# Attention with top-k masks and two expert layers: the sums and inverses of a round two rounds on, and the divides between the mask subtractions

## The chip, the cores and the metric

The kernel runs on one core of a Trainium2 chip. It uses five engines that run side by side: TensorE (PE in the profile, with its weight loads as PEld), VectorE (DVE), ScalarE (ACT), GpSimd (POOL), and SyncE (SP), which issues most DMAs. The metric is the device time of one execution in microseconds, lower is better.

## The reference

Three parts follow one another. Attention has 4 batches, 8 heads, 576 positions and head size 64. In it only the 32 largest scores of each row count. The second part is a layer of three projections whose elementwise maximum is projected back. The third sends each of the 2304 tokens to one of 8 experts.

```python
scores = scale * np.matmul(q, k.transpose(0, 1, 3, 2))
kth = np.partition(scores, -32, axis=-1)[..., -32:-31]
scores = np.where(scores >= kth, scores, -1e9)
attn = np.exp(scores - scores.max(-1, keepdims=True))
attn = attn / (attn.sum(-1, keepdims=True) + 1e-9)
x = np.matmul(attn, v)                                  # then tokens x 512
x = np.maximum(np.maximum(x @ w1, x @ w2), x @ w3) @ w_out
logits = x @ w_gate + modality_bias[modality_id]        # one expert per token
out = gate_w * (np.maximum(x @ w1[e], 0) @ w2[e])       # for the tokens of expert e
```

## The kernel before

Attention runs in 48 rounds. A round takes one pair of heads and a block of 192 queries, as three tiles of 128 rows (tiles 0 and 1 are one head each, tile 2 holds the remaining 64 rows of both). Each engine has its own program, a loop over rounds, and waits on semaphores that count the steps of the others. All queues are in order.

What happens to round r, engine by engine:
- TensorE computes its scores two rounds early, in its own round r-2: items Q0, Q1, Q2 (`score_tile`, L1324 and L1329). It transposes the probabilities in its round r+2: items H0, H1, H2 (`transpose_tile`, L1342). It multiplies them with the values in round r+3: item V (`weigh_values`, L1358). Between these stand the matmul groups of the second part (`moe_group`). The order inside a round comes from `round_items`: Q0, V, Q1, H0, half of the groups, H1, Q2, H2, the other groups. Which groups fall into which round is written out in `PARTS`, a cycle of eight rounds (one for 384 tokens), in use from round 6 on; rounds 2 to 5 have one group each that multiplies weights. Round 16 is the third of a cycle, and has a transposing group and two small products for the gate.
- ScalarE copies the scores out (`copy_scores`, L938 to L946). When `kth` is there, it makes a mask for each tile (`under`, L919, writing `below`): those of tiles 0 and 1 near the end of its round r, that of tile 2 behind the copy of Q0 in round r+1. In round r+1 it takes the exponentials and their row sums (`exp`, L927), and in round r+2 copies the transposed probabilities (`copy_probsT`, L956).
- VectorE selects the 32 largest in its round r: a chain of seven steps k = 0 to 6 of MAX8 and MATCH_REPLACE8 for each tile (L1130, L1132), and at the end `kth` (L1172). In the midst of this chain of round r it adds the sums of round r-1 (`full_sums`, L1115, behind step 5) and inverts them (`inverses`, L1120, in step 6).
- GpSimd, in its round r: subtracts the masks of round r-1 from the scores, three tiles (`leave_out`, L787); adds the two ways of the second part where a unit is finished (`add_ways`, L818); makes the key differences for round r+3 (L729); folds the scores of round r+2 (L740 to L743); multiplies the exponentials of round r-1 by the inverse sums, three tiles (`divide`, L795); and in the first rounds subtracts weights (L809).

The exponential of a tile waits for its subtraction (`masked_ready`). The transpose of a tile waits for its divide (`probs_ready`). `divide(r)` waits for `inverses(r)`.

The buffers: the probabilities and the sums have two slots, by r % 2. The scores have four, and `below` has one for each tile.

After the last round come the remaining groups. Then the tokens are listed and gathered by expert, and the experts' products follow (L1450, L1467) from about 748 us on.

Of the kernel before, what the change touches and what calls it, by code (L numbers as in the profile page):

```python
# [27 lines left out]
ROUNDS = BLOCKS * RPB  # L28
# [4 lines left out]
GROUP = 3  # L33
# [21 lines left out]
FOLDED = 2  # L55
FOLD_BUFS = 3

AFTER_Q0, AFTER_H0, AFTER_H2, AHEAD_OF_LAST = 0, 3, 7, 9
INVERSE_AT = 5
TOP_BUFS = 3  # L60
CHAIN_STEPS = CHAIN * GROUP + SMALL_CHAIN * FOLDED

# [40 lines left out]
def wait_apart(eng, passed, sem, value):  # L103


    eng.wait_ge(sem, value)
    eng.sem_inc(passed, 1)
# [53 lines left out]
def scored(r, i):  # L161


    return r * GROUP + score_order(r).index(i) + 1


def in_range(r):

    return 0 <= r < ROUNDS


def finished_units(r):

    return [(m, g[1]) for m, g in maxout_groups(r) if g[0] == "A" and g[2] == WAYS - 1]
# [227 lines left out]
def program(nc, qT, kT, v, w_in, w3T, w_out, w_gate, modality, bias, e_w1, e_w2, shared, x2_dram, list_dram, out):  # L402

    with ExitStack() as ctx:
# [311 lines left out]
        def _(pool):  # L716
# [5 lines left out]
            def key_differences(r):  # L722

                slot = r % 2
                pool.wait_ge(qk_in[slot], (r // 2 + 1) * QK_LOADS)
                if r >= 2:

                    wait_apart(pool, passed, scores_ready, scored(r - 2, 1))
                nc.gpsimd.tensor_tensor(k_diff[:, slot, :], k_sb[:, slot, 0:HALF], k_sb[:, slot, HALF:SEQ],  # L729
                                        ALU.subtract).then_inc(k_diff_ready, 1)  # L730

            def fold(r):

                slot, ring = r % FOLD_BUFS, r % RING
                wait_apart(pool, passed, scores_copied, scored(r, 1))
                if r >= FOLD_BUFS:

                    wait_apart(pool, passed, topk_step, (r - FOLD_BUFS + 1) * CHAIN_STEPS)
                second = scores[:, ring, 0:FOLDED, HALF:SEQ]
                nc.gpsimd.tensor_tensor(upper[:, slot, :, :], second, rise[:, :, :], ALU.add).then_inc(fold_step, 1)  # L740
                nc.gpsimd.tensor_tensor(lower[:, slot, :, :], second, fall[:, :, :], ALU.subtract).then_inc(fold_step, 1)  # L741
                pool.wait_ge(fold_step, r * 3 + 1)
                nc.gpsimd.tensor_tensor(scores[:, ring, 0:FOLDED, 0:HALF], upper[:, slot, :, :], fall[:, :, :],  # L743
                                        ALU.subtract).then_inc(fold_step, 1)
# [34 lines left out]
            nc.gpsimd.memset(shared.places[:, :, 1:ENTRY], 0.0)  # L779
            nc.gpsimd.iota(shared.places[:, :, 0:1].bitcast(I32), [[P, T], [0, 1]], base=0, channel_multiplier=1)  # L780

            def leave_out(r):

                for i in range(GROUP):

                    wait_apart(pool, passed, below_ready, r * GROUP + i + 1)
                    nc.gpsimd.tensor_tensor(scores[:, r % RING, i, :], scores[:, r % RING, i, :], below[:, i, :],  # L787
                                            ALU.subtract).then_inc(masked_ready, 1)

            def divide(r):  # L790

                pool.wait_ge(inverses_ready, r + 1)
                for i in range(GROUP):
                    part = probs[:, r % PROB_BUFS, i, 0:SEQ]
                    nc.gpsimd.tensor_scalar(part, part, inverse[:, r % 2, i:i + 1], 0.0, ALU.mult, ALU.add)\  # L795
                      .then_inc(probs_ready, 1)

            def weight_difference(n):

                w, c = n // DK, n % DK  # L800
                if n == 0:
                    pool.wait_ge(w_in_sem, 16 * WAYS)
                if n == DK:
                    pool.wait_ge(w3_in_sem, 16 * 2)
                if w == 1:

                    pool.wait_ge(w_differences, c + 1)
                other = w_sb[:, 1, c, :] if w == 0 else w3_sb[:, c, :]
                nc.gpsimd.tensor_tensor(w_sb[:, w, c, :], w_sb[:, w, c, :], other, ALU.subtract)\  # L809
                  .then_inc(w_differences, 1)  # L810

            def add_ways(m, u):

                n, half, first = m * UNITS + u, u // HALF_UNITS, u % HALF_UNITS * 2

                pool.wait_ge(moe_copied, PLACE[m, ("A", u, 1)] + 1)
                both = [ways[:, n % UNIT_BUFS, w, :].rearrange("p (a n) -> p a n", a=2) for w in range(WAYS)]
                nc.gpsimd.tensor_tensor(hT[:, m % 2, first:first + 2, half * BLK:(half + 1) * BLK], both[0], both[1],  # L818
                                        ALU.add).then_inc(ways_added, 1)

            for r in range(-AHEAD, LOAD_AT + 1):
                if in_range(r - 1):
                    leave_out(r - 1)
                for m, u in finished_units(r - 1):
                    add_ways(m, u)
                if in_range(r + AHEAD + 1):
                    key_differences(r + AHEAD + 1)
                if in_range(r + AHEAD):
                    fold(r + AHEAD)
                if in_range(r - 1):  # L830
                    divide(r - 1)
                if r + AHEAD < DK * WAYS:
                    weight_difference(r + AHEAD)

# [67 lines left out]
        def _(act):  # L902
# [99 lines left out]
            def one_round(r):  # L1002
# [29 lines left out]
                for _, step in steps[ran:]:  # L1032
                    step()
# [76 lines left out]
        def _(dve):  # L1110
            def full_sums(r):


                dve.wait_ge(exps_done, (r + 1) * GROUP)
                nc.vector.tensor_reduce(full_sum[:, r % 2, :], sums[:, r % 2, :, :], AX.X, ALU.add).then_inc(sum_step, 1)  # L1115

            def inverses(r):

                dve.wait_ge(sum_step, r + 1)
                nc.vector.reciprocal(inverse[:, r % 2, :], full_sum[:, r % 2, :]).then_inc(inverses_ready, 1)  # L1120

            def one_round(r):
                slot, steps = r % FOLD_BUFS, [r * CHAIN_STEPS]

                def select(k, src, dst, best, before):

                    if k > 0:
                        wait_apart(dve, passed, topk_step, before)
                    if k % 2 == 0:
                        nc.vector.max(best, src).then_inc(topk_step, 1)  # L1130
                    else:
                        nc.vector.match_replace(dst, best, src, LOWEST).then_inc(topk_step, 1)  # L1132
                    steps[0] += 1
                    return steps[0]

                def full(k, before):
                    if k == 0:

                        wait_apart(dve, passed, scores_copied, scored(r, FOLDED))
                    return select(k, scores[:, r % RING, FOLDED, :] if k < 2 else work[:, :], work[:, :],  # L1140
                                  best_eight(r, FOLDED, k // 2), before)

                upper_at, lower_at, full_at = [0] * FOLDED, [0] * FOLDED, 0
                if r == 0:
                    for k in range(CHAIN):
                        full_at = full(k, full_at)
                for k in range(CHAIN):
                    if k < 2:

                        wait_apart(dve, passed, fold_step, r * 3 + (1 if k == 0 else 3))  # L1150
                    for i in range(FOLDED):
                        part = upper[:, slot, i, :]
                        upper_at[i] = select(k, part, part, best_eight(r, i, k // 2), upper_at[i])
                        if k == INVERSE_AT + 1 and i == 0 and r >= 1:
                            inverses(r - 1)
                    if r > 0:
                        full_at = full(k, full_at)
                    if k == 0:

                        wait_apart(dve, passed, fold_step, r * 3 + 2)  # L1160
                    for i in range(FOLDED if k < SMALL_CHAIN else 0):
                        part = lower[:, slot, i, :]
                        lower_at[i] = select(k, part, part, best_eight_lower(r, i, k // 2), lower_at[i])
                    if k == INVERSE_AT and r >= 1:
                        full_sums(r - 1)

                wait_apart(dve, passed, topk_step, steps[0])
                pairs = top[:, r % TOP_BUFS, :, 0:TOP_STEP * (TOPK // 2 + 1)]
                nc.vector.tensor_reduce(smaller[:, :, :], pairs.rearrange("p i (j a) -> p i j a", a=TOP_STEP),
                                        AX.X, ALU.min).then_inc(pair_step, 1)  # L1170
                dve.wait_ge(pair_step, r + 1)
                nc.vector.tensor_reduce(kth[:, r % TOP_BUFS, :], smaller[:, :, :], AX.X, ALU.max).then_inc(kth_ready, 1)  # L1172
# [2 lines left out]
            dve.wait_ge(sum_pads_ready, 1)  # L1175
            for r in range(ROUNDS):
                one_round(r)


            link = linker(dve, early.step)  # L1180
            dve.wait_ge(ids_in, 16)
# [372 lines left out]
```

## Time and profile before

| | us |
|---|---|
| median of 3 runs | 968.61 (967.39 to 971.51) |
| the profiled execution | 970.57 |
| its span, from first to last instruction | 969.0 |
| TensorE busy (matmuls) | 908.8 |
| VectorE busy | 717.8 |
| GpSimd busy | 660.3 |
| ScalarE busy | 577.4 |
| mean granted TensorE clock | 0.990 |

A busy time is the sum over the engine's instructions. An engine that is idle waits for a semaphore, and the profile names the instruction that released it. In a timeline a row merges instructions of one line that follow one another: start in us, time in us, engine, line, operation, output and inputs, count. In brackets stands how long the engine was idle ahead of it, and for whom. Two instructions of one engine overlap a little at their ends, so a row of three is shorter than three times one.

Rounds can be told apart by TensorE's rows: each begins with Q0 (L1324 from `k_sb`), and H0 is the first row of L1342 behind the second row of L1324 (from `k_diff`).

### The profile page before, as it was taken

How to read it: one execution, taken by the hardware profiler on the slowest of the kernel's cores; microseconds unless marked ns; L12 is line 12 of the kernel's file. 1: busy time of each engine (PE TensorE's matmuls, PEld its weight loads, DVE VectorE, ACT ScalarE, POOL GpSimd, SP SyncE). 2: the span in 40 equal slices, each digit the busy share in tenths (PEclk: the TensorE clock that was granted, in tenths of full speed). 3: DMA queues.
4: the chain of work that ended last, by engine and by line, in shares of the span. 5: the costliest groups of instructions: out<-in, count | busy, mean ns of one | idle time of the engine just before them, and what ended most of it. 6: DMA issues, size and time to landing. Idle time of an engine off the chain costs nothing.

```text
span 969.0 us, 17781 instructions
## 1 busy us (share of the span) xinstructions
PE 908.8 (94%) x5132; PEld 690.2 (71%) x5133; DVE 717.8 (74%) x2191; ACT 577.4 (60%) x1226; POOL 660.3 (68%) x624
## 2 busy tenths in 40 slices
PE   4688999999999999999999999999999999999996
PEld 2354857768585776758586685957685998998895
DVE  5999999989999989999999899999503621251120
ACT  2577786777777777767777677776523321342211
POOL 7999997887988789888878879885453312231221
PEclk9999998999999999999999999999999999999998
DMA  5821121232211222121112222111043061116110
GB/s 196 253 58 46 42 59 57 58 113 55 60 44 56 68 58 67 44 68 51 49 58 57 63 58 60 53 30 46 13 145 100 18 221 56 54 38 222 43 54 32
DMA packets 69270, 70.84 MB, mean 73 GB/s; under 512 B 15456, under 2 KB 50560, under 8 KB 69184
## 3 DMA queue, kind: packets, MB, share of 16 engines
q1 hardware_dynamic: 65264, 59.44, 20.2%
q0 software_dynamic: 3920, 10.40, 3.5%
q8 instruction: 36, 0.59, 0.2%
q14 instruction: 50, 0.41, 0.1%
HBM read 59.05 MB, written 10.76 MB: 72 GB/s over the span
## 4 chain that ended last, share of the span: by engine, by line
PE 71%; issue 10%; ACT 6%; DVE 5%; POOL 3%; DMA 1%; POOLq 0%; SPq 0%; DVEq 0%; ACTq 0%
PE m_ps L1385 17%; PE m_ps L1467 10%; PE s_ps L1450 8%; PE t_ps L1342 7%; PE m_ps L1411 7%; PE o_ps L1358 5%; PE m_ps L1399 5%; PE s_ps L1324 4%; PE s_ps L1329 3%; PE o_ps L1450 3%; DVE top L1130 2%; ACT probs L927 1%; POOL dispatch_list L395 1%; PE m_ps L1418 1%; PE m_ps L1404 1%
## 5 line engine op out<-in xcount | busy, mean ns | idle before, releaser
L787 POOL TENSOR_TENSOR scores<-scores,below 128x576 f32<-128x576 f32 x144 | 200.3, 1417 | 88.0 <-ACT below L919 87.4
L1385 PE MATMUL m_ps<-xT,w_sb 128*128 128x192 f32 x1152 | 199.6, 331 | 1.2 <-ACT xT L963 1.2
L1385 PEld LDWEIGHTS m_ps<-xT,w_sb 128*128 128x128 f32 x1152 | 189.8, 193 | 1.5 <-ACT xT L963 1.5
L1130 DVE MAX8 top<-upper 128x8 f32<-128x288 f32 x384 | 159.4, 448 | 0.7 <-issue 0.6
L1132 DVE MATCH_REPLACE8 upper<-top,upper 128x288 f32<-128x288 f32 x288 | 125.3, 443 | 0.2 <-issue 0.2
L1342 PEld LDWEIGHTS t_ps<-ident,probs 128*128 128x128 f32 x720 | 80.3, 142 | 59.6 <-issue 51.1
L927 ACT ACTIVATE probs<-scores,shift 128x576 f32<-128x576 f32 x144 | 111.3, 783 | 18.3 <-issue 18.3
L956 ACT COPY probsT<-t_ps 128x640 f32<-128x640 f32 x192 | 103.4, 564 | 28.0 <-PE t_ps L1342 26.8
L1342 PE MATMUL t_ps<-ident,probs 128*128 128x128 f32 x720 | 107.4, 280 | 11.8 <-ACT probsT L956 11.8
L795 POOL TENSOR_SCALAR probs<-probs,inverse 128x576 f32<-128x576 f32 x144 | 105.4, 754 | 7.3 <-DVE inverse L1120 7.2
L919 ACT ACTIVATE below<-scores,steep_kth 128x576 f32<-128x576 f32 x144 | 106.6, 771 | 2.2
L1130 DVE MAX8 top<-work 128x8 f32<-128x576 f32 x144 | 107.1, 744 | 0.4
L864 POOL DMA_INDIRECT out_rows<-y_sb,info x18 | 17.9, 997 | 109.0 <-ACT y_sb L1056 71.9
L1358 PE MATMUL o_ps<-probsT,v_sb 128*64 128x192 f32 x960 | 88.6, 331 | 1.9 <-issue 1.5
L1411 PE MATMUL m_ps<-wo_sb,stage 128*128 128x512 f32 x192 | 85.2, 592 | 0.0
L1358 PEld LDWEIGHTS o_ps<-probsT,v_sb 128*64 128x64 f32 x960 | 65.9, 136 | 26.4 <-issue 20.2
L984 ACT ACTIVATE stage<-m_ps 128x384 f32<-128x384 f32 x72 | 35.2, 489 | 74.7 <-PE m_ps L1385 74.7
L1130 DVE MAX8 top<-lower 128x8 f32<-128x288 f32 x192 | 77.2, 445 | 0.5 <-POOL lower L741 0.5
L740 POOL TENSOR_TENSOR upper<-scores,rise 128x576 f32<-128x576 f32 x48 | 67.9, 1415 | 5.7 <-ACT fall L944 5.2
L1216 DVE SCALAR_TENSOR_TENSOR hTl<-s_ps,hTh 128x384 fp32r<-128x384 f32 x36 | 19.8, 556 | 70.1 <-ACT hTh L1048 70.1
L1132 DVE MATCH_REPLACE8 work<-top,work 128x576 f32<-128x576 f32 x96 | 71.3, 742 | 0.0
L1329 PE MATMUL s_ps<-k_sb,q_rest 128*128 128x288 f32 x192 | 59.0, 433 | 10.8 <-ACT fall L944 6.0
(208 smaller groups left out, 1789.1 us busy)
## 6 DMA issues: line engine op xcount, KB each, us to landing
k_sb<-keys_t SPq DMA_DIRECT2D x48, 288.0 KB, 2.6
v_sb<-values SPq DMA_DIRECT2D x48, 256.0 KB, 2.7
raw<-e_w SPq DMA_DIRECT2D x12, 1024.0 KB, 5.4
maxout_rows<-x_rows SPq DMA_DIRECT2D x18, 256.0 KB, 2.2
q_sb<-queries_t SPq DMA_DIRECT2D x48, 64.0 KB, 2.5
w_sb<-w SPq DMA_DIRECT2D x2, 1536.0 KB, 8.3
q_rest<-queries_t SPq DMA_DIRECT2D x96, 16.0 KB, 2.3
v_sb<-values SPq DMA_DIRECT2D x48, 32.0 KB, 2.6
```

The lines of the kernel that those rows point to most:

```text
L787: nc.gpsimd.tensor_tensor(scores[:, r % RING, i, :], scores[:, r % RING, i, :], below[:, i, :], ALU.subtract).then_inc(masked_ready, 1)
L795: nc.gpsimd.tensor_scalar(part, part, inverse[:, r % 2, i:i + 1], 0.0, ALU.mult, ALU.add)\
L919: nc.scalar.activation(below[:, i, :], scores[:, r % RING, i, :], ACT.Relu, bias=steep_kth[:, top_slot, i:i + 1], scale=-STEEP).then_inc(b ...
L927: nc.scalar.activation(probs[:, r % PROB_BUFS, i, 0:SEQ], scores[:, r % RING, i, :], ACT.Exp, bias=shift[:, top_slot, i:i + 1], scale=SCAL ...
L956: ins = nc.scalar.copy(probsT[:, h, :, row:row + rows], blocks[:, :, part:part + rows])
L1130: nc.vector.max(best, src).then_inc(topk_step, 1)
L1132: nc.vector.match_replace(dst, best, src, LOWEST).then_inc(topk_step, 1)
L1342: ins = nc.tensor.transpose(t_ps[:, c * P:(c + 1) * P], probs[:, r % PROB_BUFS, i, c * P:(c + 1) * P], ident[:, :])
L1358: ins = nc.tensor.matmul(o_ps[h * HEAD:(h + 1) * HEAD, 0:BLK], v_sb[:, slot, c, h * HEAD:(h + 1) * HEAD], probsT[:, h, c, :], start=(c == ...
L1385: ins = nc.tensor.matmul(dst[:, a * BLK:(a + 1) * BLK], w_sb[:, w, c, (first + a) * P:(first + a + 1) * P], xT[:, m % 2, c, b % SPAN * BLK ...
L1411: ins = nc.tensor.matmul(dst[:, :], hT[:, m % 2, j, i * P:(i + 1) * P], wo_sb[:, j, :], start=False, stop=(j == FB - 1))
L1450: ins = nc.tensor.matmul(h_ps[f % H_BANKS][:, 0:CH], w[:, k, f * P:(f + 1) * P], x[:, k, :], start=(k == 0 and i == 0), stop=(k == DK - 1 ...
```

## The change

VectorE takes the sums of round r-2 behind step 0 of round r and inverts them in step 1, instead of those of round r-1 in steps 5 and 6. The sums and inverses of the last round but one follow behind the loop. GpSimd divides round r-2 in its round r, between the subtractions of tiles 0 and 1 and that of tile 2, instead of dividing round r-1 at the end of round r.

```diff
-            def leave_out(r):
-                for i in range(GROUP):
+            def leave_out(r, tiles):
+                for i in tiles:
                     wait_apart(pool, passed, below_ready, r * GROUP + i + 1)
...
             for r in range(-AHEAD, LOAD_AT + 1):
                 if in_range(r - 1):
-                    leave_out(r - 1)
+                    leave_out(r - 1, range(FOLDED))
+                if in_range(r - 2):
+                    divide(r - 2)
+                if in_range(r - 1):
+                    leave_out(r - 1, range(FOLDED, GROUP))
                 for m, u in finished_units(r - 1):
                     add_ways(m, u)
                 if in_range(r + AHEAD + 1):
                     key_differences(r + AHEAD + 1)
                 if in_range(r + AHEAD):
                     fold(r + AHEAD)
-                if in_range(r - 1):
-                    divide(r - 1)
...
                         upper_at[i] = select(k, part, part, best_eight(r, i, k // 2), upper_at[i])
-                        if k == INVERSE_AT + 1 and i == 0 and r >= 1:
-                            inverses(r - 1)
+                    if k == 1 and r >= 2:
+                        inverses(r - 2)
...
-                    if k == INVERSE_AT and r >= 1:
-                        full_sums(r - 1)
+                    if k == 0 and r >= 2:
+                        full_sums(r - 2)
...
             for r in range(ROUNDS):
                 one_round(r)
-
+            full_sums(ROUNDS - 2)
+            inverses(ROUNDS - 2)
```

`FOLDED` is 2 and `GROUP` is 3, so the first call takes tiles 0 and 1 and the second tile 2. The constant `INVERSE_AT` goes.

## Rows read from the trace of the kernel before

**Rows 1.** The page, part 1: busy us, share of the span and instructions.
```profile
PE 908.8 (94%) x5132; PEld 690.2 (71%) x5133; DVE 717.8 (74%) x2191; ACT 577.4 (60%) x1226; POOL 660.3 (68%) x624
```
**Rows 2.** List of waits: us in total, times, longest us.
```profile
POOL scores L787 <- ACT below L919: 87.4, 46, 4.9
...
DVE full_sum L1115 <- ACT probs L927: 26.7, 25, 2.9
...
ACT steep_kth L910 <- DVE kth L1172: 3.0, 4, 1.0
```
**Rows 3.** Timeline of GpSimd, rounds 16 to 22.
```profile
238.94 4.15 POOL L787 TENSOR_TENSOR scores<-scores,below 128x576 f32<-128x576 f32 x3 [3.89 <-ACT below L919]
...
249.87 2.17 POOL L795 TENSOR_SCALAR probs<-probs,inverse 128x576 f32<-128x576 f32 x3
...
264.65 4.15 POOL L787 TENSOR_TENSOR scores<-scores,below 128x576 f32<-128x576 f32 x3 [1.47 <-ACT below L919]
...
292.36 4.15 POOL L787 TENSOR_TENSOR scores<-scores,below 128x576 f32<-128x576 f32 x3 [1.99 <-ACT below L919]
...
306.53 4.25 POOL L787 TENSOR_TENSOR scores<-scores,below 128x576 f32<-128x576 f32 x3 [1.09 <-ACT below L919]
...
323.95 1.41 POOL L787 TENSOR_TENSOR scores<-scores,below 128x576 f32<-128x576 f32 x1 [2.61 <-ACT below L919]
```
**Rows 4.** Timeline of TensorE: item H0 of rounds 16, 18, 20 and 21.
```profile
241.42 0.76 PE L1342 MATMUL t_ps<-ident,probs 128*128 128x128 f32 x5
...
267.13 0.77 PE L1342 MATMUL t_ps<-ident,probs 128*128 128x128 f32 x5
...
295.64 0.77 PE L1342 MATMUL t_ps<-ident,probs 128*128 128x128 f32 x5
...
310.22 0.77 PE L1342 MATMUL t_ps<-ident,probs 128*128 128x128 f32 x5
```
**Rows 5.** Timeline of ScalarE: the third exponential of round 16.
```profile
244.38 0.80 ACT L927 ACTIVATE probs<-scores,shift 128x576 f32<-128x576 f32 x1
```
**Rows 6.** Timeline of GpSimd: the subtractions of rounds 2, 9 and 10.
```profile
46.55 4.15 POOL L787 TENSOR_TENSOR scores<-scores,below 128x576 f32<-128x576 f32 x3
...
136.75 4.16 POOL L787 TENSOR_TENSOR scores<-scores,below 128x576 f32<-128x576 f32 x3
...
149.25 4.14 POOL L787 TENSOR_TENSOR scores<-scores,below 128x576 f32<-128x576 f32 x3 [0.70 <-ACT below L919]
```
**Rows 7.** Timeline of TensorE: H0 of rounds 2, 6, 9; a wait; Q1 of 10.
```profile
43.75 1.33 PE L1342 MATMUL t_ps<-ident,probs 128*128 128x128 f32 x5
...
97.84 0.77 PE L1342 MATMUL t_ps<-ident,probs 128*128 128x128 f32 x5
...
100.83 4.49 PE L1385 MATMUL m_ps<-xT,w_sb 128*128 128x192 f32 x26 [1.23 <-ACT xT L963]
...
138.12 0.77 PE L1342 MATMUL t_ps<-ident,probs 128*128 128x128 f32 x5
...
151.03 0.76 PE L1324 MATMUL s_ps<-k_diff,q_sb 64*128 64x288 f32 x4 [1.94 <-ACT scores L938]
```
**Rows 8.** Timeline of ScalarE: an exponential of round 2, the scalars of round 9.
```profile
48.06 0.78 ACT L927 ACTIVATE probs<-scores,shift 128x576 f32<-128x576 f32 x1 [5.20 <-issue]
...
147.94 0.20 ACT L910 ACTIVATE steep_kth<-kth 128x3 f32<-128x3 f32 x1 [0.96 <-DVE kth L1172]
```
**Rows 9.** Timeline of VectorE: the sums in round 1.
```profile
37.54 0.16 DVE L1115 TENSOR_REDUCE full_sum<-sums 128x3 f32<-128x6 f32 x1 [1.80 <-ACT probs L927]
```
**Rows 10.** Timeline of GpSimd: the subtractions of round 48.
```profile
686.26 4.22 POOL L787 TENSOR_TENSOR scores<-scores,below 128x576 f32<-128x576 f32 x3 [4.94 <-ACT below L919]
```
**Rows 11.** Timeline of TensorE: item H0 of round 48.
```profile
689.00 0.77 PE L1342 MATMUL t_ps<-ident,probs 128*128 128x128 f32 x5
```
**Rows 12.** Busy us by stretch; PEclk is the granted clock, behind it DMA.
```profile
151.00:159.00 8.00, 7.96 (x33) 7.61 (x34) 8.00 (x25) 4.62 (x12) 7.24 (x6) 0.57 0.06 16
492.00:498.00 6.00, 6.00 (x33) 5.93 (x32) 5.90 (x19) 3.86 (x11) 6.00 (x6) 0.72 0.05 14
```

More of the change, by code:

```diff
@@ L58 @@
 AFTER_Q0, AFTER_H0, AFTER_H2, AHEAD_OF_LAST = 0, 3, 7, 9
-INVERSE_AT = 5
 TOP_BUFS = 3
```

## The prediction

> **What bounds the kernel now.** I read the page first, then the list of waits, then the timelines of GpSimd, TensorE and ScalarE side by side. The page gives TensorE 94% busy, VectorE 74%, GpSimd 68%, ScalarE 60% [rows 1]. The span has three parts. Up to about 147 us VectorE's selection, 13.35 us a round and almost without waits, and GpSimd's queue set the pace. From there to 709 us TensorE's own queue does: in most rounds its matmuls stand back to back. After that come the last projections and the experts, which the change does not touch.
>
> The waits that look like a prize are those of the edited lines: VectorE waits 26.7 us in 25 rounds at `full_sums` for the last exponential of the round before. GpSimd waits 87.4 us for ScalarE's masks ahead of its subtractions. But who waits for VectorE in turn? ScalarE waits for `kth` only 4 times, 3.0 us in all [rows 2]. A round of VectorE without its stall is 13.35 us; the eight TensorE rounds of a cycle (238 to 350 us) take 14.0 us each. So VectorE's stalls are slack it would otherwise spend elsewhere.
>
> **The change, part by part.** *Sums and inverses.* The same two small instructions a round stand at another place; they cost 0.16 us each in both [rows 9], so their work is priced at nothing. Their wait goes: in round r the exponentials of r-2 are long done. What is late next on VectorE is nothing that ScalarE waits for. The exception is the start: two stalls stand there, 1.80 us [rows 9] and one more of 1.1, and `kth` of rounds 3 to 9 comes 2.9 us earlier. This is worth something only where ScalarE waits for `kth`: 0.96 us in round 9 [rows 8].
>
> *Divides.* Before, `divide(r-1)` ends GpSimd's round r, and TensorE transposes its result in round r+1, several us later. In round 16 the three divides stand at 249.87 and take 2.17 us [rows 3]. After, `divide(r-2)` is issued in round r, behind the subtractions of tiles 0 and 1 of round r-1, and TensorE transposes it in the same round r (item H0, the fourth of the round). So H0 can start no sooner than the first subtraction plus two subtractions (4.15/3 = 1.38 us each, 2.77) plus one divide (2.17/3 = 0.72) plus the handover. For the handover I take 0.15: the first subtraction of rows 6 ends at 46.55 + 1.38 = 47.93 and ScalarE's exponential, which waited, starts at 48.06 [rows 6, 8]. Sum 3.65 us. The first subtraction itself waits for ScalarE's mask, which sits in ScalarE's queue near the end of TensorE's round before; so it cannot move ahead, and shifts with TensorE.
>
> That gives a test for each round: the distance from the first subtraction to H0 in the trace of before must be 3.65 us, or TensorE waits for the rest.
> - Round 16: 238.94 to 241.42, 2.48: short by 1.1 [rows 3, 4].
> - Round 17: its subtractions are bound by GpSimd's queue, whose total of work is the same; the shift of round 16 covers it: 0.
> - Round 18: 264.65 to 267.13, 2.48: short by 1.1 [rows 3, 4].
> - Round 20: 292.36 to 295.64, 3.28: short by 0.4 [rows 3, 4].
> - Round 21: 306.53 to 310.22, 3.69: just enough. Rounds 19 and 23 are like it or better [rows 3, 4].
> - Round 22: the divides fall into the 2.61 us in which GpSimd waits for the third mask [rows 3], 2.17 of work in 2.61 of waiting: hidden wholly. This is what the edit fits.
>
> So one cycle of eight rounds costs 1.1 + 1.1 + 0.4 = 2.6 us, and TensorE has no slack behind it to take it back. The cycle stands four times in full (rounds 16 to 47): 10.4 us. Round 12 has the distance of round 20: 0.4. Rounds 47 and 48 have too little as well: 686.26 to 689.00 [rows 10, 11] is short by 0.9, the other by 0.7: 1.6. Together 12.4.
>
> *The third subtraction* now comes 2.17 us later where no wait covers it, and ScalarE's third exponential waits for it. In round 16 that exponential started at 244.38 [rows 5]; now 238.94 + 4.15 + 2.17 = 245.26, 0.9 later, which is inside the 1.1 that H0 already costs. Behind it stand the copies that TensorE's H2 waits for, so if H0 were not late this would cost the 0.9 instead. The adds of the two ways, the key difference and the fold come 2.2 us later too; the fold of round 18 would end at 252, against ScalarE's next use of its buffers at 254.7: covered.
>
> *The start.* In round 2 the divides are no longer done at 43, ahead of the subtractions of 46.55, but behind two of them. GpSimd reaches these 2.2 us earlier (44.4), so the first divide ends at 47.9 and H0 of round 2 moves from 43.75 to 48.05: 4.3 us [rows 6, 7]. In rounds 3 to 6 a closed ring then runs: H0 and weight product 5.8, H1 and Q2 1.6, copy, scalars and mask 2.5, then the 3.65 above: 13.55 us a round, against (97.84 - 43.75)/4 = 13.5 before [rows 7]. So the 4.3 stays. Round 6 adds some 1.3 for a slower start-up of the first matmuls and the ring, and gives back 1.2, since TensorE's wait for `xT` goes [rows 7]: 4.3. Round 8 costs 0.4 more. In round 9 the subtractions are bound by GpSimd's queue: 136.75 + 4.3 + 3.65 = 144.7 against H0 at 138.12, 6.6, which is 2.0 more. In round 10 the 0.96 of `kth` is gained [rows 8], and 149.25 to H0 at 151.03 + 0.69 = 151.72, 2.47, is short by 1.2 [rows 6, 7]. Total of the start: 4.3 + 0.4 + 2.0 - 0.96 + 1.2 = 6.9. Its bounds: 0, if the waits that TensorE already has there absorb it, and 9.
>
> *The clock.* TensorE's granted clock averages 0.57 from 151 to 159 us [rows 12]: most of it at the lower of its two levels (1.2 of 2.4 GHz), just behind an idle time of 1.94 us [rows 7] and in a run of transposes and 8-column products. That costs 8.0 x 0.43 = 3.4 us. Round 34 has a fall of 6.0 x 0.28 = 1.7 us at the same place of the cycle [rows 12], behind a wait half as long; rounds 18, 26 and 42 have the same wait and no fall. The change adds 1.1 us idle exactly there. Bounds: nothing, or a fall of 3.4 in all four, 13.6 - 1.7 = 11.9 more than now. I take 3.4, one full fall more: the waits then come to 2.0 us together, which is near the row of 1.94, but only one of five such places has paid the full price.
>
> Sum: 12.4 + 6.9 + 3.4 = 22.7 us. The profiled execution took 970.57 us around a span of 969.0, 2 us above the median of 968.61. On it that is 993; on the median 991.
>
> **Rivals.** *A, the start is free.* TensorE waits often before 150 us, and VectorE comes 2.9 us earlier there. If the delay is absorbed and the clock stays as it is: 968.6 + 12.4 = 981. Against it: the waits in rounds 3 to 6 are waits for the same GpSimd queue.
>
> *B, the clock falls in every round like 18.* 968.6 + 12.4 + 6.9 + 11.9 = 1000. For it speaks round 10, against it rounds 26 and 42, which kept the clock.
>
> *C, the other side: VectorE's lead is passed on.* The mechanism is the removed wait at `full_sums` only: `kth` earlier, ScalarE's masks earlier, the subtractions earlier, and H0 covered. It decides from the point at which the first subtraction comes 1.2 us earlier in rounds 16 and 18. If only the start gains, 968.6 - 2.9 = 966; the whole 26.7 would make 942. Against it: ScalarE issues the mask in order, behind TensorE's last copies, and did not wait for `kth` there [rows 2]. A page of the Trainium skill would have it otherwise: Perfetto Trace Analysis, section "Identifying the Most-Contended Engine", says that matmul busy time is a poor measure, that TensorE is to be judged by weight loads, and that one should improve the engine with the highest occupancy. By that rule TensorE has 71%, VectorE 74% and is the one to free, and the change would gain. Rows 1 has both numbers; the back-to-back matmuls of rounds 19 to 23 speak against the rule here.
>
> *D, no difference*: the waits at H0 fall where TensorE would have waited anyway (0.61 at Q1, 0.42 at H1 and 0.95 at H2 in round 16), and the sum is within 4 us: 970. Against it: these waits have their own cause, ScalarE's queue, which the late H0 also pushes back.
>
> **How the numbers follow.** Forecast 0.58, A 0.14, B 0.16, C 0.06, D 0.06. The time is that of the forecast, 991. Its own range is 984 to 998 (start 3 to 9, clock 0 to 7). The range goes down towards A and up over B: 979 to 1003. A measurement of this kernel can tell 0.5%, 5 us. Faster 0.06 (C), within 0.5% 0.06 (D), slower 0.88.
>
> **What would show it.** In the changed profile: waits of VectorE at `full_sum` nearly gone; GpSimd's idle time ahead of the subtractions less by about what the divides fill; a new row "TensorE transposes wait for GpSimd `probs`", some 1.1 us in rounds 16, 18 and their likes, and 2 us or more in rounds 2 to 9; H0 of round 10 near 158.5 instead of 151.7; the granted clock below 1 behind the transposes of rounds 18, 26, 34 or 42. I am wrong if that row is missing or small, or if `kth` turns out to have held TensorE, so that rounds 16 and 18 get shorter.

## The result: 2.5% slower, and the profile after

The changed kernel takes 993.95 us (median of 4 runs, 993.76 to 994.21), the kernel before 970.06 (4 runs, 967.39 to 971.51). The ratio is 1.025, interval 1.0223 to 1.0277. The forecast was 991 in a range of 979 to 1003. In the profiled executions the span (first to last instruction) went from 969.0 to 992.4 us, 23.4 more, and the mean granted clock of TensorE from 0.990 to 0.982.

The page's part 1 after, which answers to [rows 1]:
```profile
PE 917.5 (92%) x5132; PEld 696.5 (70%) x5133; DVE 720.9 (73%) x2191; ACT 582.5 (59%) x1226; POOL 657.7 (66%) x624
```
The instruction counts are unchanged. TensorE is busy 8.7 us longer for the same instructions: its granted clock was lower. The rest of the 23.4 is idle time.

The list of waits after (us in total, times, longest us), which answers to [rows 2]:
```profile
POOL scores L786 <- ACT below L920: 124.0, 46, 9.3
...
DVE full_sum L1116 <- ACT probs L928: 45.2, 33, 4.4
...
PE t_ps L1344 <- POOL probs L794: 25.4, 23, 5.8
PE s_ps L1326 <- ACT scores L939: 15.6, 19, 1.4
```
The third row is new: TensorE's transposes wait for GpSimd's divides. The fourth is a wait ahead of Q1, which comes back below with the clock. The first two grew, 87.4 to 124.0 and 26.7 to 45.2, where I had both shrinking. No row has ScalarE waiting for `kth` any more.

TensorE's timeline after (start us, length, then in brackets the idle time before and what ended it): item H0 of rounds 2, 9, 10, 16, 18, 20 and 48, with Q1 of rounds 16 and 18.
```profile
48.43 0.87 PE L1344 MATMUL t_ps<-ident,probs 128*128 128x128 f32 x3 [5.77 <-POOL probs L794]
...
145.85 1.33 PE L1344 MATMUL t_ps<-ident,probs 128*128 128x128 f32 x5 [1.82 <-POOL probs L794]
...
162.25 0.77 PE L1344 MATMUL t_ps<-ident,probs 128*128 128x128 f32 x5 [1.00 <-POOL probs L794]
...
248.25 0.76 PE L1326 MATMUL s_ps<-k_diff,q_sb 64*128 64x288 f32 x4 [0.61 <-ACT scores L939]
250.02 0.89 PE L1344 MATMUL t_ps<-ident,probs 128*128 128x128 f32 x5 [1.02 <-POOL probs L794]
...
276.61 0.76 PE L1326 MATMUL s_ps<-k_diff,q_sb 64*128 64x288 f32 x4 [0.89 <-ACT scores L939]
278.37 0.77 PE L1344 MATMUL t_ps<-ident,probs 128*128 128x128 f32 x5 [1.01 <-POOL probs L794]
...
307.16 0.77 PE L1344 MATMUL t_ps<-ident,probs 128*128 128x128 f32 x5 [0.22 <-POOL probs L794]
...
714.38 0.77 PE L1344 MATMUL t_ps<-ident,probs 128*128 128x128 f32 x5 [0.83 <-POOL probs L794]
```
In rounds 16 and 18 H0 had no wait before [rows 4]; now it has about 1.0 us in each and 0.22 in round 20.

GpSimd's timeline after, rounds 16 and 22 (compare [rows 3]):
```profile
246.45 2.79 POOL L786 TENSOR_TENSOR scores<-scores,below 128x576 f32<-128x576 f32 x2 [3.97 <-ACT below L920]
249.21 2.20 POOL L794 TENSOR_SCALAR probs<-probs,inverse 128x576 f32<-128x576 f32 x3
251.36 1.42 POOL L786 TENSOR_TENSOR scores<-scores,below 128x576 f32<-128x576 f32 x1
...
330.09 2.77 POOL L786 TENSOR_TENSOR scores<-scores,below 128x576 f32<-128x576 f32 x2 [0.85 <-ACT below L920]
332.84 2.19 POOL L794 TENSOR_SCALAR probs<-probs,inverse 128x576 f32<-128x576 f32 x3
335.49 1.41 POOL L786 TENSOR_TENSOR scores<-scores,below 128x576 f32<-128x576 f32 x1 [0.46 <-ACT below L920]
```
Round 22 is the fit that the edit suggests: 2.19 us of divides stand where 2.61 of waiting stood, and 0.46 are left. Round 16 is where it hurts. From 246.45 to H0's start at 250.02 are 3.57 us, and TensorE had room for 2.48.

How far the changed kernel lags behind the kernel before, at the start of each round's first score product (us after less us before, from the two timelines of TensorE):
```
round   3     9     10     11    16    17     19     21     25
lag    4.65  5.84  10.52  7.23  7.52  10.16  11.24  11.53  12.51
round  27     29     33     35     37     41     43     45
lag   16.92  17.21  18.56  17.95  18.24  19.24  23.65  23.93
```
The lag grows in steps, each in a round in which H0 waits. Between the steps it stays the same. It shrinks twice from round 9 on, in rounds 10 and 34: there the clock fell in the kernel before and not in the changed one. Some steps are larger than their wait (4.41 us in round 26, 0.98 in round 24). These are falls of the clock, seen in busy us by stretch after (engines PE, PEld, DVE, ACT, POOL, then the granted clock and DMA), which answers to [rows 12]:
```profile
144.00:152.00 8.00, 6.18 (x13) 3.33 (x13) 7.82 (x27) 4.29 (x10) 8.00 (x8) 0.57 0.02 7
248.00:256.00 8.00, 6.73 (x30) 5.78 (x31) 5.24 (x18) 6.23 (x14) 8.00 (x9) 0.66 0.14 38
392.00:400.00 8.00, 7.17 (x30) 7.09 (x31) 7.82 (x27) 3.87 (x11) 8.00 (x9) 0.62 0.08 24
480.00:488.00 8.00, 6.09 (x48) 5.04 (x45) 5.04 (x13) 6.96 (x17) 7.34 (x8) 0.88 0.13 38
488.00:496.00 8.00, 8.00 (x42) 4.74 (x43) 7.92 (x28) 6.08 (x15) 8.00 (x7) 0.91 0.21 52
624.00:632.00 8.00, 6.99 (x31) 6.54 (x29) 7.82 (x27) 4.51 (x12) 8.00 (x9) 0.62 0.12 35
```
Up to the end of attention five falls (rounds 9, 16, 26, 32, 42) stand against two before (rounds 10 and 34).

Behind round 45 the lag first grows by the waits of rounds 47 and 48, to 25.39 us where the last projections begin (709.67 before, 735.06 after). Then it shrinks, to 23.40 when the experts' products are under way (757.00 and 780.40). TensorE's wait for gathered rows and the first split of them is 0.44 us shorter. The other 1.55 are a fall of the clock that only the kernel before has. Before:
```profile
748.00:752.00 4.00, 3.39 (x13) 3.30 (x13) 1.76 (x8) 0.17 (x1) 0.00 (x0) 0.63 0.00 0
```
After, the same products:
```profile
772.00:776.00 4.00, 3.45 (x24) 3.33 (x23) 1.98 (x9) 0.75 (x2) 0.00 (x0) 1.00 0.01 4
```

### The profile page after: what moved, and what is told of

It reads as the page before. It is cut to its first block, busy times and chain, and to the rows that moved or that the text cites. A ratio compares the mean times of both kernels' runs of the same rounds, so it can differ in the third digit from the quotient of the medians.

```text
span 992.4 us, 17781 instructions
## 1 busy us (share of the span) xinstructions
PE 917.5 (92%) x5132; PEld 696.5 (70%) x5133; DVE 720.9 (73%) x2191; ACT 582.5 (59%) x1226; POOL 657.7 (66%) x624
## 4 chain that ended last, share of the span: by engine, by line
PE 71%; POOL 8%; issue 8%; ACT 6%; DVE 1%; DMA 1%; POOLq 0%; DVEq 0%; ACTq 0%
PE m_ps L1387 15%; PE m_ps L1469 10%; PE t_ps L1344 8%; PE s_ps L1452 7%; PE m_ps L1413 7%; PE m_ps L1401 5%; PE s_ps L1331 4%; PE o_ps L1360 4%; POOL scores L786 4%; PE s_ps L1326 3%; PE o_ps L1452 3%; POOL probs L794 2%; PE m_ps L1396 2%; ACT below L920 2%; ACT probsT L957 2%
## 5 line engine op out<-in xcount | busy, mean ns | idle before, releaser
L786 POOL TENSOR_TENSOR scores<-scores,below 128x576 f32<-128x576 f32 x144 | 201.3, 1413 | 124.0 <-ACT below L920 124.0
L1131 DVE MAX8 top<-upper 128x8 f32<-128x288 f32 x384 | 156.3, 449 | 0.3 <-issue 0.3
L1344 PE MATMUL t_ps<-ident,probs 128*128 128x128 f32 x720 | 109.7, 284 | 31.8 <-POOL probs L794 25.4
L1344 PEld LDWEIGHTS t_ps<-ident,probs 128*128 128x128 f32 x720 | 82.9, 145 | 79.7 <-issue 42.8
L1413 PE MATMUL m_ps<-wo_sb,stage 128*128 128x512 f32 x192 | 87.5, 605 | 0.0
L1331 PE MATMUL s_ps<-k_sb,q_rest 128*128 128x288 f32 x192 | 61.0, 444 | 10.7 <-ACT fall L945 6.1
```

The lines of the kernel that those rows point to most:

```text
L1331: ins = nc.tensor.matmul(s_ps[:, half, 0:HALF], q_rest[:, slot, :], k_sb[:, slot, half * HALF:(half + 1) * HALF], start=True, stop=True)
L1344: ins = nc.tensor.transpose(t_ps[:, c * P:(c + 1) * P], probs[:, r % PROB_BUFS, i, c * P:(c + 1) * P], ident[:, :])
L1413: ins = nc.tensor.matmul(dst[:, :], hT[:, m % 2, j, i * P:(i + 1) * P], wo_sb[:, j, :], start=False, stop=(j == FB - 1))
```

## The experiments

The changed loop was written with two functions that say, for each round q, whether its divides and its sums stand at the new place. A ratio, and a difference with a sign, is against the kernel before on the same chip. The expectations give times as they would be beside a kernel before of about 970 us; on the chips of E1 to E4 and E5 to E8 it took 974.02 and 972.93, so they are compared here by the difference. `q` is the round whose divides or sums are meant, and `r % 8` the rest of a round's number divided by 8. The edits are shortened. The experiments' kernels have other line numbers: L798, L806, L942, L1130 and L1363 are the subtraction, the divide, the exponential, the sums and the transpose.

**Which half costs: the divides alone (E1).**
```
 divide_late(q): True      # as in the change
-sums_late(q): True
+sums_late(q): False       # full_sums, inverses one round on, as before
```


> The divides stand where the change puts them (behind two subtractions, a round later); the sums and inverses stay in steps 5 and 6 of the next round, as before. Theory (TensorE waits for the first divide at H0; VectorE's stall costs nothing): as the changed kernel, 992 to 996 us, with TensorE's waits for GpSimd's divides again 25 us and VectorE's wait at the sums back at about 27 to 30 us. Rival C (VectorE's lead is worth something, and only the divides hide it): 3 us or more above the changed kernel, 997 or more.

Measured: 999.19 us (998.01 to 1002.97) against 974.02 (970.65 to 976.05), ratio 1.0276 (1.0243 to 1.031), 25.2 more. By the difference, 22 to 26 were expected and 27 or more by rival C. The lag is that of the change (7.40 at round 11, 24.1 at 45), with a fall of the clock in round 24 instead of 26. The waits of E1:
```profile
DVE full_sum L1130 <- ACT probs L942: 50.9, 41, 4.5
...
PE t_ps L1363 <- POOL probs L806: 23.9, 23, 4.1
```
The loss sits in the divides. The move of the sums gives nothing that shows in the time (rival C): the change's own 23.9 lies within E1's interval. The wait at `full_sum`, which I expected near that of before, is 50.9, a miss. It is 24.2 us more than before, and the lag at round 45 is 24.1: VectorE's own work is the same, so its waits take up what the rounds are longer. This last is argued from the two numbers.

**Where it costs: the start as before (E2), the short rounds as before (E3), both (E4).** "Short rounds" are those that the test of the prediction found short: r % 8 in 0, 2, 4, and 47, 48.
```
-divide_late(q): True
+divide_late(q): q >= 9                                                  # E2
+divide_late(q): q < 9 or (q < 45 and (q + 2) % 8 not in (0, 2, 4))       # E3
+divide_late(q): 9 <= q < 45 and (q + 2) % 8 not in (0, 2, 4)             # E4
 sums_late(q): the same
```


> Sums and divides of rounds 0 to 8 as before, those of round 9 and later as in the change. Theory: the start costs 7 us of its own, so 987 us (986 to 988). Rival A (the start is free): 994.

> As the change, but the divides and sums that rounds 12, 16, 18, 20 and their likes, 47 and 48 would take (the rounds whose distance from the first subtraction to H0 is under 3.65 us) stand as before; the start as in the change. Theory: the waits at H0 of these rounds go, 10.3 + 1.3 = 11.6 us, and with them the clock's falls in rounds 16, 26, 32 and 42, net 6.5 us: 976 us (974 to 978). If the falls of the clock don't hang on these waits: 982.

> Late divides and sums only in the rounds from 11 to 46 whose distance is 3.65 us or more (those like 11, 13, 14, 15, 17); all others as before. Theory: the late place costs nothing where the distance is there and gains nothing either, since VectorE's stall is not waited for: 970 us, as before (968 to 972). Rival C: the stalls it removes are worth some us: 966 or less. Another rival, that a late divide costs something in every round (through the third exponential or the fold): 975 or more.

Measured, on the chip of E1:
```
E2  991.36 (990.59 to 992.28)  ratio 1.0186 (1.0163 to 1.021)   +17.3   lag +0.16 at round 11, +16.8 at 45
E3  982.45 (978.29 to 983.26)  ratio 1.0086 (1.0053 to 1.012)    +8.4   lag +7.25 at round 11, the same to 34
E4  972.98 (968.87 to 975.66)  ratio 0.9982 (0.9963 to 1.0001)   -1.0   lag constant at +0.5 to round 34
```
The change less E2 is 6.6 to 7.9 us (23.9 or E1's 25.2, less 17.3): the start costs its computed 6.9, and rival A falls. E3 and E4 show the other side of the test: in rounds with 3.65 us or more between the first subtraction and H0 the new place costs nothing. E3's 8.4 is a little over the 4 to 8 expected and under the 12 of its rival. Its trace says why: the falls of rounds 16, 26 and 32 went with the waits, but in round 42 the clock fell as well (0.57 from 612 to 616 us) with no wait at H0, behind 1.05 us at Q1. E4 keeps the move in 23 of the rounds, with sums and divides, and gains nothing either: its interval reaches 1.0001.

**The distance itself: divides behind one subtraction (E5), behind three (E6), ahead of all (E7).** The change puts them behind two.
```
-leave_out(r - 1, range(2)); divide(r - 2); leave_out(r - 1, range(2, GROUP))
+leave_out(r - 1, range(1)); divide(r - 2); leave_out(r - 1, range(1, GROUP))   # E5
+leave_out(r - 1, range(3)); divide(r - 2)                                      # E6
+divide(r - 2); leave_out(r - 1, range(GROUP))                                  # E7
```


> As the change, but the divides stand behind the first subtraction of the round instead of the second. H0 then needs 1.38 + 0.72 + 0.15 = 2.3 us from the first subtraction, less than the 2.48 of rounds 16 and 18; the second and third exponential come 2.17 us later instead of the third alone. Theory: no waits for the divide at H0 in the steady rounds; the late exponentials push H2 by 0.9 us in round 16 and 0.4 in round 18, so 1.3 us a cycle instead of 2.4, and the start costs some 5: about 12 us over before with one or two falls of the clock more than before, 10 to 16 over before on the same chip. If the exponentials cost nothing, 5 to 8 over before.

> As the change, but the divides stand behind all three subtractions. The exponentials are as early as before; H0 needs 3 x 1.38 + 0.72 + 0.15 = 5.0 us from the first subtraction, which no steady round has (2.48 to 3.96). Theory: short by 2.5, 2.5, 1.0, 1.7, 1.3, 1.4 and 1.3 us in the rounds of a cycle, some 12 us a cycle, and some 12 in the start: 50 to 75 us over before. If it were the late third exponential that cost the time in the change, this one would be near before (0 to 5 over).

> Sums and inverses as in the change (two rounds on); the divides of round r-2 stand ahead of the first subtraction of round r, which is where they stood before but for the weight differences of the first rounds. So it is the move of the sums alone. Theory: GpSimd waits for the masks there and has the time, H0 is as early as before, VectorE's lead is not waited for but in round 9: 0 to 1 us under before. Rival C: 3 us or more under before. VectorE's wait at the sums is not gone but stands at the next bound, the exponentials of two rounds before: 30 us or more.

Measured, on a chip where the kernel before took 972.93 (968.66 to 975.46, 17 runs):
```
E5   978.76 (976.02 to 979.51)    ratio 1.0065 (1.0044 to 1.0085)    +5.8
E6  1081.63 (1080.63 to 1083.32)  ratio 1.113  (1.111 to 1.1151)   +108.7
E7   970.91 (968.56 to 974.29)    ratio 0.9987 (0.9972 to 1.0002)    -2.0
```
In E5 H0 of round 16 needs 2.2 us (1.40 to the divide, 0.75 for it, 0.06 for the handover) and has 2.48, so it no longer waits. What remains is the second path that I had computed for the late exponentials. GpSimd's timeline in E5, round 16:
```profile
238.33 1.42 POOL L798 TENSOR_TENSOR scores<-scores,below 128x576 f32<-128x576 f32 x1 [3.99 <-ACT below L934]
239.73 2.19 POOL L806 TENSOR_SCALAR probs<-probs,inverse 128x576 f32<-128x576 f32 x3
241.88 2.77 POOL L798 TENSOR_TENSOR scores<-scores,below 128x576 f32<-128x576 f32 x2
```
ScalarE's timeline in E5, the same round, exponentials of tiles 1 and 2:
```profile
243.41 0.78 ACT L942 ACTIVATE probs<-scores,shift 128x576 f32<-128x576 f32 x1 [0.27 <-POOL scores L798]
...
244.77 0.78 ACT L942 ACTIVATE probs<-scores,shift 128x576 f32<-128x576 f32 x1 [0.49 <-POOL scores L798]
```
TensorE's timeline in E5, item H2 of the same round:
```profile
246.91 0.74 PE L1363 MATMUL t_ps<-ident,probs 128*128 128x128 f32 x5 [1.93 <-ACT probsT L971]
```
H2 waits 1.93 us for ScalarE's copies, where it waited 0.95 before: the lag steps by 0.98 in round 16 and 0.32 in round 18. So the two paths are real and stand beside each other; in the change the longer one (H0) counts. I expected 10 to 16 us in all and missed: E5's start costs nothing net (lag -0.6 at round 11), and its profile has no more falls than the kernel before (that of round 34 stands in round 32).

E6 has the sign and the mechanism and misses in size. Its wait for the divides:
```profile
PE t_ps L1363 <- POOL probs L806: 87.8, 47, 7.4
```
It waits 47 times instead of 23, and the steady waits are near the computed ones (2.37 us in rounds 16 and 18, 1.26 in 17, 1.58 in 20). The lag is 27.5 us at round 11 and 98.9 at 45, where I expected 50 to 75 in all. The start, for which I had some 12, repeats the ring with a wait of 2.84 us in each of rounds 3 to 6. And thirteen falls of the clock came up to round 45, for which I had nothing.

E7 takes the divides out of the way, and only the sums are late. The wait at `full_sum` is 21.0 us there (26.7 before; I expected 30 or more, a miss), and the time is that of before within its interval. This is the direct test of rival C: the moved sums alone are worth 0.9987 (0.9972 to 1.0002). By the rule of the Trainium skill, page Perfetto Trace Analysis, section "Identifying the Most-Contended Engine", VectorE (74% against 71% of weight loads) is the engine to optimize first. E7 gives no support for that: making VectorE's stall 5.7 us shorter brought nothing that can be told from noise, and before the change ScalarE waited for `kth` only 3.0 us in all. E7 takes no work from VectorE, so what less work there would bring, no run here shows.

**Is the rest the clock? (E8, E9, E10).** Two products of 288 columns whose result nobody reads, 0.97 us together, are added on TensorE. They fill the idle time. E8 is the changed kernel with them ahead of H0 in rounds r % 8 of 0 and 2; E9 the kernel before with them ahead of Q1 in rounds r % 8 of 2, all from round 10 to 43; E10 is E7 with them at the places of E9 and in round 6.
```
+for _ in range(2):
+    nc.tensor.matmul(t_ps[:, 640:640 + HALF], q_rest[:, slot, :], k_sb[:, slot, 0:HALF],
+                     start=True, stop=True)
```


> The changed kernel with two more matrix products (of 288 columns, 0.97 us together, into a part of PSUM that nobody reads) ahead of H0 in the rounds 10, 16, 18, 24, 26, 32, 34, 40 and 42, where TensorE waits 1.0 us for the divide. The products sit in the wait. Theory (these waits bring the clock down): the falls of rounds 16, 26, 32 and 42 go or get fewer and the time is 4 to 10 us under the changed kernel, so 14 to 20 us over before instead of 24. If the clock falls for another reason: the time of the changed kernel, or up to 1 us more.

> The kernel before with two unused matrix products (0.97 us together) ahead of Q1 in rounds 10, 18, 26, 34 and 42, where TensorE waits 0.9 us (1.9 in round 10) for ScalarE's copy. If such waits, behind few real products, bring the clock down, its falls in round 10 and at times in round 34 or its likes go: 3 to 5 us under before, with less spread between runs. If not: before, or up to 0.5 us more.

> Sums two rounds on and divides ahead of the subtractions (as in the run of the front place), and the same two products ahead of Q1 in rounds 6, 10, 18, 26, 34 and 42. If both small gains add up: 1 us from VectorE's lead and 3 to 5 from the clock, 4 to 6 us under before, the fastest of all. If the lead is worth nothing: as the filled kernel before.

Measured (E8 on the chip of E5 to E7; E9 and E10 on a chip where the kernel before took 967.36, 963.14 to 970.54, 22 runs):
```
E8   989.72 (986.38 to 992.78)  ratio 1.0173 (1.0155 to 1.0192)  +16.8
E9   965.11 (963.79 to 968.41)  ratio 0.9986 (0.9969 to 1.0003)   -2.3
E10  964.81 (963.62 to 966.35)  ratio 0.9976 (0.9962 to 0.9991)   -2.6
```
The stretches around the falls of the change, busy us by engine and granted clock, of the changed kernel:
```profile
240.00:264.00 24.00, 22.37 (x133) 17.08 (x131) 21.23 (x68) 18.01 (x40) 19.37 (x18) 0.86 0.18 47
384.00:408.00 24.00, 22.11 (x126) 18.82 (x126) 23.64 (x77) 15.25 (x34) 15.07 (x14) 0.86 0.19 58
616.00:640.00 24.00, 22.10 (x125) 18.73 (x124) 23.82 (x78) 15.06 (x33) 15.05 (x14) 0.86 0.19 58
```
The same stretches of E8:
```profile
240.00:264.00 24.00, 21.94 (x149) 15.99 (x148) 21.24 (x67) 18.96 (x43) 20.02 (x19) 1.00 0.17 47
384.00:408.00 24.00, 23.11 (x165) 18.98 (x163) 23.64 (x73) 19.35 (x43) 18.45 (x18) 1.00 0.25 70
616.00:640.00 24.00, 23.11 (x165) 19.74 (x162) 22.83 (x74) 18.94 (x42) 19.75 (x19) 1.00 0.22 67
```
And H0 of round 16 in E8, with the two products in its wait (one row with others of the line):
```profile
248.60 0.76 PE L1345 MATMUL s_ps<-k_diff,q_sb 64*128 64x288 f32 x4 [0.61 <-ACT scores L953]
249.29 1.24 PE L1447 MATMUL t_ps<-k_sb,q_rest 128*128 128x288 f32 x4
250.37 0.76 PE L1363 MATMUL t_ps<-ident,probs 128*128 128x128 f32 x5
...
255.39 0.74 PE L1363 MATMUL t_ps<-ident,probs 128*128 128x128 f32 x5 [1.45 <-ACT probsT L971]
```
With the wait filled, H0 starts no later against its round and the clock stays at 1.00 at these places. In E8 the lag goes from 7.58 at round 11 to 15.85 at 45 in steps of 0.97, 1.08 and 0.28, with one of 1.26 in round 32 (the change waits 1.29 us there too, without the filler) and one of -0.61 in round 34, 1.08 less the fall that only the kernel before has. That separates the terms: 8.3, plus 1.7 for that fall, makes 10.0 us for the waits; the change itself has 23.93 - 7.23 = 16.7, so 6.7 are the clock. At round 45 the change lags 8.1 us more than E8. The times say 7.1 (23.9 less 16.8), on two chips. E8's 16.8 lies in the 14 to 20 expected.

E9 and E10 were aimed at a version that beats both kernels. E10 does, by 2.6 us, 0.24%, with an interval that ends just below 1 (0.9991); 4 to 6 were expected. E9, the kernel before with the filler alone, lies within 0.3 us of E10, so nothing shows that the new order adds to the filler. E9's own interval includes 1, and 3 to 5 were expected. In its profile the falls of rounds 10 and 34 are gone and the lag at round 45 is -3.5, but around the start of the experts' products stands a fall of 3.4 us (740 to 752), where the kernel before had 1.7. Its 12 runs form two groups, seven of 963.8 to 965.2 at a mean clock of 0.997 or 0.998 and five of 967.5 to 968.4 at 0.994 or 0.995, and the profiled one is of the slower group. The filler does not make the best run faster: the kernel before had one of 963.14. By the profiles it takes away falls, and by the times those come only in some runs.

## Why the prediction was right, and where it was off

- **The mechanism** (H0 no sooner than the first subtraction + two subtractions + one divide + handover) was right. The distance was 3.57 us in round 16 against 3.65 computed (the handover is 0.06, not 0.15); the waits are 1.02, 1.01 and 0.22 us in rounds 16, 18, 20 against 1.1, 1.1, 0.4. (3.65 less 2.48 is 1.17, which the prediction rounded down.) Rounds 17, 19, 21 and 23 don't wait for the divides, as computed.
- **Steady waits:** 10.8 predicted for the four cycles and round 12, 10.0 by E8, of which round 12 gave 0.3 (0.4 predicted). Rounds 47 and 48 wait 0.49 + 0.83 = 1.3 (1.6 predicted), and the lag grows by 1.5 from round 45 to the last projections.
- **The start:** 6.9 predicted, 7.2 measured, and E2 takes it away. H0 of round 2 came at 48.43 (48.05). Single rounds were less exact, and that their sum fits is in part luck. At the start of round 9 the lag was 5.84 where the terms give 4.7: rounds 3 to 5 added 1.9 and round 6 gave back 1.0, where I had next to nothing. Round 9 gave 1.8 of its 2.0, round 10 -0.1 against 0.2, and the fall of round 9 cost some 0.4 less than the one in round 10 before. H0 of round 10 came at 162.25, not near 158.5, because the clock fell in round 9 rather than in round 10; at round 11 this had cancelled. The sign "2 us or more in rounds 2 to 9" failed: H0 waited 5.77 us in round 2, 1.49 in rounds 3 to 6, not at all in round 7, 0.22 in round 8 and 1.82 in round 9.
- **The third exponential** of round 16 starts at 252.89, less the lag of 7.51 is 245.38, against 245.26 computed. That it lies inside H0's wait, and would cost its 0.9 if H0 were in time, is what E5 showed (0.98).
- **The clock is the term that was mis-sized:** "I take 3.4, one full fall more"; up to round 45 it was 6.7, inside the bounds of 0 and 11.9. I had looked for falls only in rounds like 18. Rounds 16 and 32, which wait 0.61 at Q1 and 1.02 and 1.29 at H0, fell too. The rows bear two readings of a fall: by the granted clock those of rounds 16, 26, 32 and 42 lose 3.4 + 3.4 + 1.7 + 3.4 = 11.9, against 1.7 before, 10.2 more; by the lag only 6.7. (With the fall behind attention that only the kernel before has, the next item, the whole execution lost 5.1 to the clock.) The falls of rounds 26 and 42 moved the lag by their full 3.3 beyond the wait, that of round 16 by 1.7 and that of round 32 by 0.1. In rounds 16 and 32 of E8, where no fall came, H2 waited 1.45 and 1.46 us for ScalarE's copy, and so it did in rounds 24 and 40 of the change, which had no fall; in rounds 16 and 32 of the change, with the fall, H2 waits for nothing. The slower transposes ran in time that would have been waiting.
- **Behind the queries,** in the last projections and the experts, I had nothing. The changed kernel gains 2.0 us there: 1.55 because the clock fell at the start of the experts' products in the kernel before and not in the changed one, and 0.44 by a shorter wait. E9 has a fall there too, E10 has none. Why the changed kernel had none in this run is open.
- **The sum:** 7.2 + 10.0 + 6.7 + 1.5 - 2.0 = 23.4, against 22.7. The close hit of the total hides errors of opposite sign: 3.3 too little for the clock of attention, 2.0 of gain that I hadn't foreseen, and 0.9 too much for the steady waits and the end.
- **Wrong: VectorE's wait at `full_sum` "nearly gone".** It is 45.2 us. What was one cause (the sums ask for exponentials of the round just before) went; but VectorE, which nobody waits for, runs ahead of a TensorE that is slower now, until it meets the exponentials of r-2 instead. The row after, in TensorE's round 16, which is VectorE's round 17 (r-2 is 15):
```profile
253.79 0.16 DVE L1116 TENSOR_REDUCE full_sum<-sums 128x3 f32<-128x6 f32 x1 [2.51 <-ACT probs L928]
```
A wait that is slack has the size of the slack: it doesn't go away with its cause.
- **Wrong: GpSimd's idle time ahead of its subtractions "less".** In round 16 it went from 3.89 [rows 3] to 3.97, because the divides left the queue ahead of it; that the whole slower round adds to it is likely and not tested. Only in rounds like 22 did the divides fill waiting time.
- **Rivals:** A fell by E2, C by E7 and E1, D by the new row of 25.4 us. B (falls in every round like 18) is half true: rounds 26 and 42 fell, 18 and 34 did not, and up to round 45 the clock's cost (6.7) lies between the forecast's 3.4 and B's 11.9.

## What to carry to other kernels

Before work is moved into another engine's idle gap, measure for every kind of round the distance from where the gap's predecessor starts to where the consumer stands in the same round; the place is free where that distance holds the work and costs exactly the shortfall elsewhere (E3, E4, E5). A stall on an engine that nobody waits for is slack, however high it stands in the list of waits; taking away its cause brought no time (E7), and in the change it reappeared larger. Price a new TensorE wait of about 1 us among transposes and small products at more than its length (here 10.0 us of waits came with 6.7 us of clock), and try the version with the wait filled. Before a total is called a hit, split it by stretch: here a fall of the clock in the kernel before, in a part that the change doesn't touch, hid a quarter of what the clock had cost elsewhere.

## What the hardware showed that I had not expected

- **A wait of 1 us can cost a clock fall of more than its length.** With waits of 0.61 and 1.02 us 0.8 us apart (round 16), 1.04 and 0.85 (round 26) or 0.89 and 1.01 (round 42), the granted clock went to 0.62 to 0.66 over 8 us, which is mostly the lower level, 1.2 of 2.4 GHz. With 0.89 and 1.01 in round 18 and 0.61 and 1.00 in round 24 it did not fall, and in E3 it fell in round 42 behind a single wait of 1.05.
- **Products that compute nothing can save time.** With 0.97 us of them in the wait, no fall stood at any of the filled places of E8; E10, also filled, had a mean granted clock of 0.998 and 1.00 from 100 to 700 us. The gain is sure only where the waits were new (E8); in E10 it is 0.24%.
- **The kernel before differs by chip:** medians of 974.02, 972.93 and 967.36 on three chips, and up to 7.4 us between runs on one. E7's 2.0 us with 12 runs against 17 stayed inside the noise; E10's 2.6 with 11 against 22 stand just outside it. A part of the difference between the chips has a place: in the profiles of E1 to E8, taken where the kernel before has the two higher medians, TensorE waits 4.0 us once in the last projections, and a fall of the clock of 1.7 or 3.4 us follows. E7's row:
```profile
731.55 3.41 PE L1425 MATMUL m_ps<-wo_sb,stage 128*128 128x512 f32 x4 [3.99 <-ACT stage L986]
```
  The profiles of both kernels of the result, E9 and E10 have no such wait. What holds ScalarE up there is not shown, and no profile of the kernel before was kept on those chips.
- **On GpSimd the subtraction of two 128x576 tiles takes 1.41 us, the "divide", a multiplication by one inverse per partition, 0.75.** So E5 (one subtraction ahead of the divides) and the change (two) differ by 1.4 us at H0.
